# Loading feed-forward weights in place, fourteen small products ahead of a loop, and a new order at the end of the first attention phase

## The reference, cut to what matters

```python
def _attn_ref(q, k, v, alpha):          # (4, 8, 768, 48) each
    for t in range(S):
        state = alpha[:, :, t, :, None] * state + np.einsum('bhd,bhe->bhde', k[:, :, t], v[:, :, t])
        y[:, :, t] = np.einsum('bhd,bhde->bhe', q[:, :, t], state)

def _moe_ref(x, U, V, w_ch1, w_ch2):    # x (4, 768, 384), rank 32, w_ch1 384 x 1536
    h = x.transpose(0, 2, 1) @ U @ V
    u = x + h.transpose(0, 2, 1)
    return u + np.maximum(u @ w_ch1, 0.0) @ w_ch2

def _moe2_ref(x, w_in, w_spatial, b_spatial, w_out):
    h = np.maximum(x @ w_in, 0.0)
    u, v = h[..., :d_ff // 2], h[..., d_ff // 2:]
    v_n = (v - mean(v)) / np.sqrt(var(v) + 1e-06)
    v_s = np.einsum('ts,bsd->btd', w_spatial, v_n) + b_spatial[None, :, None]
    return (u * v_s) @ w_out
```

## Time and profile before

| | us |
|---|---|
| median of 3 executions | 726.85 (726.44 to 726.87) |
| the profiled execution | 727.21 |
| span of its trace | 725.0 |
| PE busy, weight loads apart | 696.3 (96%) |
| DVE busy | 392.6 (54%) |
| ACT busy | 340.2 (47%) |
| POOL busy | 212.0 (29%) |

### The profile page before, as it was taken

How to read it: one execution, slowest core, us unless ns; L and a number is a source line. 1 busy time by engine, 2 the same in 40 slices (tenths; PEclk the granted TensorE clock), 3 DMA queues, 4 the chain that set the end, 5 groups by cost and what they waited for, 6 DMA issues and landing times.

```text
span 725.0 us, 25711 instructions
## 1 busy us (share of the span) xinstructions
PE 696.3 (96%) x11336; PEld 660.6 (91%) x11336; DVE 392.6 (54%) x666; ACT 340.2 (47%) x575; POOL 212.0 (29%) x143
## 2 busy tenths in 40 slices
PE   2689999999999999999999999999999999999998
PEld 2688989899899999999999999999998998999998
DVE  6888665545654654655453415125834852871671
ACT  5887654554654454556444332335532432532422
POOL 6704660410450320351220330461360060043022
PEclk9879999999999999999999999999999999999999
DMA  9415410410401221401100341011110101101001
GB/s 360 169 47 168 163 42 8 154 47 10 149 3 46 80 79 46 156 3 47 37 3 3 101 151 66 33 38 62 65 45 23 66 23 43 65 0 65 0 0 65
DMA packets 16524, 49.48 MB, mean 68 GB/s; under 512 B 1616, under 2 KB 9552, under 8 KB 15920
## 3 DMA queue, kind: packets, MB, share of 16 engines
q1 hardware_dynamic: 16432, 48.09, 18.8%
HBM read 38.65 MB, written 9.44 MB: 66 GB/s over the span
## 4 chain that ended last, share of the span: by engine, by line
PE 92%; ACT 3%; DVE 2%; issue 1%; DMA 1%; SPq 0%; DVEq 0%; ACTq 0%
PE HB L906 25%; PE ZB L994 7%; PE ZB L996 7%; PE ZB L995 7%; PE SB L906 6%; PE SB L782 5%; PE SB L1031 5%; PE ZB L906 4%; PE SB L888 2%; PE SB L1035 2%; PE ZB L1031 2%; PE ZB L1044 2%; PE SB L897 2%; PE SB L843 2%; PE SB L1044 2%
## 5 line engine op out<-in xcount | busy, mean ns | idle before, releaser
L1556 DVE SCALAR_TENSOR_TENSOR hid_lo<-HB,hid_hi 128x384 fp32r<-128x384 f32 x92 | 51.2, 556 | 139.7 <-ACT hid_hi L1238 139.3
L1238 ACT ACTIVATE hid_hi<-HB 128x384 fp32r<-128x384 f32 x92 | 45.3, 492 | 158.6 <-PE HB L906 158.5
L994 PE MATMUL ZB<-hid_hi,w2h 128*128 128x384 f32 x288 | 98.2, 341 | 0.0
L906 PE MATMUL HB<-uh,w1h 128*128 128x384 f32 x276 | 97.8, 354 | 0.2 <-DVE ul L1552 0.2
L996 PE MATMUL ZB<-hid_lo,w2h 128*128 128x384 f32 x288 | 96.5, 335 | 0.0
L995 PE MATMUL ZB<-hid_hi,w2l 128*128 128x384 f32 x288 | 96.3, 334 | 0.0
L906 PE MATMUL HB<-ul,w1h 128*128 128x384 f32 x276 | 92.5, 335 | 0.0
L906 PE MATMUL HB<-uh,w1l 128*128 128x384 f32 x276 | 92.4, 335 | 0.1
L1085 ACT COPY Qd<-Q 48x768 f32<-48x768 f32 x84 | 73.1, 871 | 12.8 <-POOL Q L674 4.3
L731 POOL TENSOR_TENSOR gl<-gf,gh 128x384 fp32r<-128x384 f32 x32 | 33.5, 1048 | 144.1 <-ACT gh L1278 143.8
L674 POOL TENSOR_TENSOR Q<-Q,bk 112x768 f32<-112x768 f32 x14 | 25.6, 1827 | 162.7 <-ACT Qd L1085 162.7
(11 more groups left out here) (269 smaller groups left out, 1516.5 us busy)
## 6 DMA issues: line engine op xcount, KB each, us to landing
Q<-in_q SPq DMA_DIRECT2D x8, 768.0 KB, 6.1
AL<-in_al SPq DMA_DIRECT2D x7, 768.0 KB, 4.5
K<-in_k SPq DMA_DIRECT2D x7, 768.0 KB, 4.2
Vt<-in_v SPq DMA_DIRECT2D x8, 576.0 KB, 3.6
mid<-x2s SPq DMA_DIRECT2D x8, 576.0 KB, 3.7
x<-mid SPq DMA_DIRECT2D x4, 1152.0 KB, 5.4
out<-o_sb SPq DMA_DIRECT2D x24, 192.0 KB, 1.8
x2s<-in_w SPq DMA_DIRECT2D x9, 384.0 KB, 5.1
```

Source lines behind the costliest of these rows:

```text
L906: last = nc.tensor.matmul(dst, weights(x, w), moving(y, m), start=(n == 0 and x == y == 0), stop=(n == total - 1 and y == 1))
L994: nc.tensor.matmul(bank, w2h[:, i, cols], hi, start=(i == 0), stop=False)
L1238: nc.scalar.activation(hid_hi[:, i % HID, :], up_bank(i)[:, 0:TILE], ACT.Relu).then_inc(h_hi, 1)
L1556: nc.vector.scalar_tensor_tensor(hid_lo[:, i % HID, :], up_bank(i)[:, 0:TILE], 0.0, hid_hi[:, i % HID, :].bitcast(F32), ALU.max, ALU.subtr ...
```

## The change

- **Weights.** w1 is loaded in three transfers of 768 KB straight into the place of its rest part (`w1f` over `w1l`), w2 in three into `w2f` over `w2l`; the rests overwrite the raw values. `x2s` no longer holds pieces, `early` is gone, w2's two parts change places (the side workspace's K now lies over `w2h`). SP waits for each load before the next: K of g = 1, V of both groups, the first third of w1, ident, U and V, the rest of w1, w2, and only then decay, keys, queries and values of batch 1. POOL's first splits of w2 wait for the KV product of g = 1 as well.
- **Spare products.** Ahead of the loop over levels PE runs 14 products of 32 x 32 on a zeroed tile; their result is overwritten.
- **Order at the phase's end.** ACT takes the copies of turned K for g = 1 ahead of the copies of its level 7 scores (`ACT_LAST`), and the first two weight pieces after them. DVE copies the squares of g = 0 behind its level 7 scaling and those of g = 1 behind the turned keys of g = 0, where both stood ahead of level 7. The third bank of turned keys for g = 1 is ZB0 where it was ZB2.
- **Halves.** Y of the first batch is computed in two halves of 64 positions a chunk, where it was one product of 128.

```diff
+SPARE = 14
-HIGH1 = {(1, T_STEP): [0, 1], (0, KV_STEP): [2, 3], (0, Y_STEP - 1): [4], (1, Y_STEP - 1): [5]}
+HIGH1 = {(1, LEVELS - 1): [0, 1], (0, KV_STEP): [2, 3], (0, Y_STEP - 1): [4], (1, Y_STEP - 1): [5]}
+ACT_LAST = [(0, MASKED), (1, MASKED), (0, LEVELS - 1), (1, T_STEP), (1, LEVELS - 1)]
...
-        side_space.SB, side_space.TB, side_space.KVB, side_space.YB = ZB, HB + ZB[2:], HB[1], ZB
+        side_space.SB, side_space.TB, side_space.KVB, side_space.YB = ZB, HB + ZB[:1], HB[1], ZB
...
-            for n in range(STAGE):
-                load_piece(n)
+            sp.wait_ge(ld_k[GROUPS - 1], 16)
             for g in range(GROUPS):
                 load_values(0, g)
-            sp.dma_start(ident[:, :], ident_d).then_inc(ld_ident, 16)
-            sp.dma_start(U_sb[:, :, :], u_w).then_inc(ld_uv, 16)
-            sp.dma_start(V_in[:, :], v_w).then_inc(ld_uv, 16)
-            for n in range(STAGE, W1_PIECES):
-                load_piece(n)
+                sp.wait_ge(ld_v[g], 16)
+            for d in range(DB):
+                sp.dma_start(w1f[:, d, :], w1[:, d, :]).then_inc(ld_w1, 16)
+                sp.wait_ge(ld_w1, 16 * (d + 1))
+                if d == 0:
+                    sp.dma_start(ident[:, :], ident_d).then_inc(ld_ident, 16)
+                    sp.dma_start(U_sb[:, :, :], u_w).then_inc(ld_uv, 16)
+                    sp.dma_start(V_in[:, :], v_w).then_inc(ld_uv, 16)
+                    sp.wait_ge(ld_ident, 16)
+                    sp.wait_ge(ld_uv, 32)
+            for n in range(0, F1B, W2_LOAD):
+                sp.dma_start(w2f[:, n:n + W2_LOAD, :], w2[:, n:n + W2_LOAD, :]).then_inc(ld_w2, 16)
+                sp.wait_ge(ld_w2, 16 * (n // W2_LOAD + 1))
             load_decay(1, 0, False)
...
             pool.wait_ge(tot_ready[0], 2 * (LEVELS - 1))
+            pool.wait_ge(aux_done[GROUPS - 1], AUX_KV)
...
+            def spare_products():
+
+                zeros = main_space.Ad[0:ROWS, 0, :, :].rearrange("p h t -> p (h t)")
+                for _ in range(SPARE):
+                    nc.tensor.matmul(main_space.SB[1][0:BLOCK, 0:BLOCK], zeros[:, 0:BLOCK], zeros[:, BLOCK:2 * BLOCK],
+                                     start=True, stop=True)
...
-                            for t in (WHOLE if first else QUARTERS) if c else []:
+                            for t in (HALVES if first else QUARTERS) if c else []:
...
+            pe.wait_ge(zeroed_s, 1)
+            spare_products()
             pe.wait_ge(zeroed_s, 4)
             with pe.Fori(0, MASKED) as n:
...
-            for g, n in LAST_STEPS:
+            for g, n in ACT_LAST + [s for s in LAST_STEPS if s not in ACT_LAST]:
...
-                if (g, n) == (1, MASKED):
-                    for h in range(GROUPS):
-                        square_copies(h, QUARTERS[2:])
+                if (g, n) == (0, LEVELS - 1):
+                    square_copies(0, QUARTERS[2:])
                 if (g, n) == (0, T_STEP):
                     key_copies(g)
+                    square_copies(1, QUARTERS[2:])
```

More of the change, by code:

```diff
@@ L87 @@
 W2_PIECES = F1B * DM // PIECE
-NW1 = W1_PIECES + W2_PIECES
+W2_LOAD = 2 * F1B // W2_PIECES
 HS = NT // 2
@@ L268, in build @@
         x2s, o = place("x2s", [P, QT, DB * TILE], o)
[L269 to L270 removed]
         at_w1 = o
         w1h, o = place("w1h", [P, DB, FF1], o, F32R)
+        w1f, _ = place("w1f", [P, DB, FF1], o)
         w1l, o = place("w1l", [P, DB, FF1], o, F32R)
[L274 removed]
+        w2f, _ = place("w2f", [P, F1B, DM], o)
+        w2l, o = place("w2l", [P, F1B, DM], o, F32R)
+        at_w2h = o
         w2h, o = place("w2h", [P, F1B, DM], o, F32R)
[L276 to L277 removed]
         at_u = o
@@ L394, in build @@
         ld_x2 = sem("ld_x2")
-        ld_piece1 = [sem(f"ld_piece1{i}") for i in range(STAGE)]
-        ld_early = [sem(f"ld_early{i}") for i in range(STAGE)]
+        ld_w1 = sem("ld_w1")
+        ld_w2 = sem("ld_w2")
         zeroed_q = [sem(f"zeroed_q{g}") for g in range(GROUPS)]
@@ L454, in build, with cut, loaded @@
         stored = [sem(f"stored{i}") for i in range(2)]
-        def cut(src, hi, lo, n):
-            flat = [x.rearrange("p a b -> p (a b)") for x in (src, hi[:, :, :], lo[:, :, :])]
+        def cut(raw, hi, lo, n):
+            flat = [x[:, :, :].rearrange("p a b -> p (a b)") for x in (raw, hi, lo)]
             return [tuple(x[:, i * PIECE:(i + 1) * PIECE] for x in flat) for i in range(n)]
[L461 to L467, removed]
+        first = cut(w1f, w1h, w1l, W1_PIECES)
+        WEIGHTS1 = first[0::2] + first[1::2] + cut(w2f, w2h, w2l, W2_PIECES)
+        def loaded(n):
+            if n < W1_PIECES:
+                return ld_w1, 16 * (n % DB + 1)
+            return ld_w2, 16 * ((n - W1_PIECES) // 2 + 1)
         nc.disable_value_cache = True
@@ L614, in _ @@
             sp.wait_ge(ld_k[0], 32)
-            for n in range(W1_PIECES, W1_PIECES + STAGE):
-                load_piece(n)
             load_queries(1, 0, False)
@@ L620, in _ @@
             sp.wait_ge(ld_v[0], 32)
-            for n in range(W1_PIECES + STAGE, NW1):
-                load_piece(n)
             for b in range(BATCH - 1):
@@ L1204, in split_high @@
             def split_high(n):
-                where, loaded, value = slot(n)
-                act.wait_ge(loaded, value)
-                nc.scalar.copy(WEIGHTS1[n][1], where).then_inc(w_hi, 1)
+                act.wait_ge(*loaded(n))
+                raw, hi, _ = WEIGHTS1[n]
+                nc.scalar.copy(hi, raw).then_inc(w_hi, 1)
             def x2_high(b, first):
```

28 lines of the change are left out of this document (9 added, 19 removed).

## The result

The changed kernel takes **735.35 us** (median of 6 runs, 731.16 to 737.17) beside 726.86 (726.44 to 727.78) for the kernel before: a ratio of 1.0091 on record, with a 95% interval of 1.0064 to 1.0117. It is slower by 0.9%. (The quotient of the two medians is 1.0117. The forecast was 725.7, the range 723.8 to 727.6. The profiled execution took 735.79 us with a span of 733.6.

What follows compares the result with a forecast made beforehand. PE and DVE were taken as nearly equal bounds of batch 0's attention phase. DVE's earlier `xu` start (0.5) plus less waiting behind it (0.6) made 1.1 us off 726.85, forecast 725.7, range 723.8 to 727.6.

Steps and rivals of the forecast that it cites:

- PE is busy to the end, so the gain is kept: Behind batch 0's attention phase: later work moves earlier with the phase's end, keeping the whole 1.1 us gain.
- they cost nothing: The 14 spare products ahead of the level loop run near 2 us, where PE waits for keys, so are free.
- The hole: PE's 1.83 us stop at 37.26 us, in group 1's level 6, goes; worth 1.0 us on PE.
- The first-round packet: Boundary moved about 3 instructions ahead of the loop's end, crossed in round one; its packet arrives 18 us before needed.
- Rival C: Packet comes late in the loop's first round, second round starts 3.8 us later; 729.6 us, chance 0.09.
- rivals B and E: B: boundary not moved into the loop, 726.4 us, chance 0.06. E: loop rounds fetch again, 744 us, chance 0.02.
- Rival A: Unbroken level 6 keeps PE's clock at 1.00, level 7 ends at 40.4 and 42.1; 724.4 us, chance 0.32.
- DVE is next: DVE becomes the late engine at the first phase's end, starting the rest of `xu` at 62.75 instead of 63.28.
- the prediction's own sign: Wrong if the phase ends over 2 us earlier at low clock, or first up product is later than 69.7 - 0.3.
- Halves: Batch 0's Y in halves takes 1.5 us a group, was 2.3; PE gains 1.6 us for two groups.
- Weights in place, and the queries: Serialized loads cost nothing: decay lands at 54.3, queries at 62.7, hidden with 2.4 us to spare.
- Rival D: Batch 1's queries land after 65.1 us, when ACT wants them, leaving no gain; 726.8 us, chance 0.06.

Runs made afterwards that it cites:

- e2: Kernel before with only 34 small filler products (136 PE instructions) added behind batch 0's token mixing; 734.92 us, ratio 1.0085.
- e1: Changed kernel with 30 small filler products behind batch 0's token mixing, making the code shift 256 instructions; 729.46 us, ratio 1.0032.
- f4: Changed kernel with 34 small filler products behind batch 0's token mixing, making the code shift 272 instructions; 729.85 us, ratio 1.0029.
- f1: Kernel before, unchanged, run and traced a second time; 725.32 us.
- g4: Changed kernel, run and traced once more without alteration; 737.58 us.
- g2: Kernel before, unchanged, run and traced a further time; 728.45 us.
- e4: Changed kernel without the 14 spare products, code shift 80 instructions; 731.48 us, ratio 1.0052.
- e3: Changed kernel with Y of the first batch computed whole again, code shift 56 instructions; 730.27 us, ratio 1.0053.
- g3: Changed kernel with whole Y and 50 small filler products behind batch 0's token mixing, code shift 256 instructions; 729.13 us, ratio 1.0030.
- f2: Changed kernel with 3 small filler products behind batch 0's token mixing, code shift 148 instructions; 735.30 us, ratio 1.0061.
- f3: Changed kernel without batch 2's group 0 loads of decay, queries and values (stale data, semaphores raised); 733.31 us, ratio 1.0070.

## Why the prediction was wrong

**The step that failed** stands at the end of the part on DVE: "PE is busy to the end, so the gain is kept". With it went the sentence on the spare products, "they cost nothing". I had counted the packets' boundaries to find where the 14 products put the one at the loop's end, and used this count for that one alone. The same shift, and the halves' 80 instructions on top, move all 70 boundaries behind. In the trace of before none of them, behind the phase, left PE idle for over 0.3 us; in after, four did. That was worth +8.1 us. Neither the halves (1.6 us on PE, no more cost thought of) nor the range had a term for it. e2 shows it without any other part of the change, e1 takes it away with all parts in place. The prediction had what was needed: the distance of 256, the price of one such stop ("from request to resumption, 3.5 us"), and the list of long waits of PE. Counting 136 forward would have put a boundary 59 instructions ahead of the longest wait of batch 1. That the packet would then be asked for only behind the wait, and that loads would delay the other three, stood in none of its rows.

**The hole.** Right in kind: the boundary was moved ahead of the loop's end, level 6 was unbroken, level 7 started when DVE was through. Wrong in its place: the packet came not in the first round, near 17 us, but in the last ones (30.6 to 35.4), and once (f4) too late. The first-round packet that the prediction looked for is another one; it fell at 13.6 with the keys' load. Rival C (a late packet in the first round) did not come about; what looked like it is chance that before has as well. Nor did rivals B and E: the hole is gone, and in the trace of after no packet of PE's code runs between 14.50 and 35.39 us, while the loop goes round.

**The clock.** Rival A's number and not the forecast's: level 7 took 1.61 us a group at the upper clock in after. The forecast had 2.6 to 2.8. A's reason does not hold: the clock was not kept up by an unbroken level 6. The loop and most of level 6 ran at the slow pace in after, and the clock came up at 39.09. In f1, with the hole, it was up for the first group of level 7 as well. In g4 its first group took 2.77 again at 0.50 and the phase ended no later (69.74 against 69.83): a low clock of 3.4 us there cost nothing that shows, with DVE as the bound.

**DVE is next.** Right, and more so than forecast. DVE came to the recurrence at 50.37 (forecast 49.9) with the loop's end 1.4 us late, and started the rest of `xu` at 63.24 (forecast 62.75). PE waited 1.62 us for it with [DVE xu_sb] as the releaser. Against g2, PE was 4.2 us ahead at token mixing and 2.0 at the first up product. By the prediction's own sign (a first up product later than 69.4) the phase counts as wrong too, at 69.83; from the loop's end it is 33.2 us, 1.3 less than in the trace that the sum was made on, near the forecast's 1.1. Since f1, without the change, has 33.3, that agreement may be luck.

**Halves.** Mis-sized: 1.84 us to run, and 1.94 from start to start in after (1.66 or 1.67 in e1, e4, f4 and g4), where I took 1.5 between bounds of 1.15 and 2.3. In e3, with Y whole, the first up product came at 69.47, no later than with halves. They bring nothing in this place and cost 80 instructions of shift.

**Weights in place, and the queries.** The chain held: decay issued at 53.5, keys landed at 62.2 and queries at 66.4, where I had 62.7. The copy of Q on ACT started at 66.41 and waited 0.81 us for them. Rival D's mechanism was there at this small price; part of the lag is the loop's late end.

**The base.** The sum was made against one trace, and that one was among the lucky ones: side keys at 14.64 where most traces have 15.7 to 16.1. I read its 10.5 us as the load's time.

What stays open: why e1 and g3, with one or two small stops (0.54 to 0.56 us) and a first phase 0.7 to 1.8 us better than g2's, have medians 1.6 us above before's. Their traced executions are under their medians (728.41 of 729.46 in e1). Without those of 738.63 and 738.10, runs of e1, e3, f2 and f4 spread over 5.9 to 10.3 us, those of before beside them over 3.8 to 4.8. f2, whose trace has four stops, also has an execution of 726.39. So stops that only some executions have are likely, but no trace was taken of a long execution of e1 or g3. No version here beat the kernel before.

## What to carry to other kernels

Any edit that adds or removes instructions on an engine that is busy to the end moves all its later code-packet boundaries. Before calling such an edit free, place the boundaries anew and look at two spots: where one falls shortly ahead of a long wait (59 and 71 instructions were too few here, 179 enough) with little but short products left of the packet behind the wait, and where one falls among large loads while the engine uses up a packet in 4 us or so. If a kernel gets slower with nothing slower in it, look for "issue" idle time in the middle of runs of like instructions, and undo the shift with filling before undoing the change. And take the base of a sum from two or three traces: between three traces of the unchanged kernel the side keys' landing moved by 1.4 us, the hole by 0.9 and DVE's scaling by 1.9, as much as the change was forecast to bring.

## What the runs showed that I had not expected

- From the end of a wait to PE's going on behind a boundary took 3.5 us in after: 1.0 to the packet's start (94.63 to 95.65), 1.0 for its 16 KB, and 1.4 until PE resumed (96.68 to 98.10). The other three stops ended 1.2 to 1.35 us behind the landing. The packets of these three, crossed 0.1 to 1.4 us behind the issue of a 576 or 768 KB load, started 2.9 to 3.85 us behind the crossing; without the loads (f3) it was 1.0.
- The Trainium skill, "Runtime: NRT & Kernel Launch", section "Instruction fetch mechanics", calls the crossing of a 16 KiB boundary "mostly hidden". Of some 70 boundaries most are hidden here too, but four were not and left PE idle for 5.2 us, and the low clock behind one cost 2.5 more.
- A stop of 1.88 us can bring the clock down for 6.8 us, which costs more than the stop (2.5 us). In g4 one of 2.16 brought it down for 3.4 us, one of 2.73 for 6.8. Those of 1.31 and 1.02 us in after left it at 1.00, and so did one of 1.81 in e2.
- In 12 of 13 traces in which a code packet fell into the end of the side keys' load the keys landed at 15.7 to 16.1 us, with a single part of sixteen 1.1 us behind the others in after and 1.6 in g2, and the whole load waits for it. In f1 it fell there too and no part was late. That the packet delays the part is a guess; no run took it apart.
